# Pooled attention and two feed-forward layers: the first batch in plain fp32 with one order of stages per engine, two buffers for q, x0 loads two places later

## The reference

```
q, k, v: (8, 8, 576, 64)                       # batch, heads, sequence, head size
k_p, v_p = mean of 8 neighbouring keys, values  # 72 of each
attn = softmax(q @ k_p.T / 8)                  # 576 x 72 for each head
x0 = (attn @ v_p), heads side by side           # 4608 x 512
h = x0 @ w1_in;  g = max(0.01 h, h);  x1 = g @ w1_out     # 512 -> 2048 -> 512
h = x1 @ w2_in;  g = h * clip(h + 3, 0, 6) / 6;  out = g @ w2_out
```

## Time and profile before

| | |
|---|---|
| runs, us | 1729.87, 1733.42, 1739.12 (median 1733.42) |
| the profiled execution, us | 1732.34 |
| its span, us | 1730.6 |
| mean granted clock of TensorE | 0.992 |
| busy: PE, DVE, ACT, POOL | 98%, 59%, 37%, 23% |
| DMA | 366.83 MB, mean 212 GB/s |

### The profile page before, as it was taken

How to read it: one execution, slowest core, us unless ns; L and a number is a source line. 1 busy time by engine, 2 the same in 40 slices (tenths; PEclk the granted TensorE clock), 3 DMA queues, 4 the chain that set the end, 5 groups by cost and what they waited for, 6 DMA issues and landing times. The chain is left out here.

```text
span 1730.6 us, 33189 instructions
## 1 busy us (share of the span) xinstructions
PE 1691.3 (98%) x10588; PEld 1506.7 (87%) x10588; DVE 1024.0 (59%) x1807; ACT 632.5 (37%) x1329; POOL 394.1 (23%) x427
## 2 busy tenths in 40 slices
PE   7999999999999999999999999999999999999999
PEld 6788888988888888899999888989898888989898
DVE  7767776686766867666454655454544444444444
ACT  4554443333333433333222333333333333333332
POOL 6226542021120212103332202121211112121200
PEclk8999999999999999999999999999999999999999
DMA  7756877667676676767777757575757675757562
GB/s 199 228 159 201 271 249 247 214 201 259 204 243 220 208 247 215 242 196 268 239 258 245 257 172 224 176 220 175 218 170 220 178 219 171 223 173 223 173 197 77
DMA packets 215810, 366.83 MB, mean 212 GB/s; under 512 B 22464, under 2 KB 47040, under 8 KB 215744
## 3 DMA queue, kind: packets, MB, share of 16 engines
q1 hardware_dynamic: 215744, 366.04, 67.3%
HBM read 308.28 MB, written 57.67 MB: 211 GB/s over the span
## 5 line engine op out<-in xcount | busy, mean ns | idle before, releaser
L1416 PE MATMUL ps_h<-xs_hi,ring 128*128 128x256 f32 x3808 | 823.8, 285 | 20.5 <-ACT p L1045 15.9
L1416 PEld LDWEIGHTS ps_h<-xs_hi,ring 128*128 128x128 f32 x3808 | 645.5, 190 | 69.5 <-ACT p L1045 19.8
L1416 PE MATMUL ps_h<-xs_lo,ring 128*128 128x256 f32 x1904 | 537.4, 282 | 0.0
L1416 PEld LDWEIGHTS ps_h<-xs_lo,ring 128*128 128x128 f32 x1904 | 361.2, 190 | 27.0
L931 ACT ACTIVATE g_hi<-gate 128x512 fp32r<-128x512 f32 x288 | 181.9, 632 | 404.6 <-DVE gate L1126 221.8
L1185 DVE TENSOR_TENSOR u<-ps_h,p 128x256 f32<-128x256 f32 x272 | 114.2, 420 | 205.9 <-PE ps_h L1416 155.0
L1369 PE MATMUL ps_y<-g_hi,wout_hi 128*128 128x512 f32 x576 | 229.2, 398 | 0.5 <-DVE y_stage L1181 0.3
L1370 PE MATMUL ps_y<-g_lo,wout_hi 128*128 128x512 f32 x576 | 228.7, 397 | 0.0
L1370 PE MATMUL ps_y<-wout_lo,g_hi 128*128 128x512 f32 x576 | 227.8, 395 | 0.0
L1369 PE MATMUL ps_y<-wout_hi,g_hi 128*128 128x512 f32 x576 | 227.5, 395 | 0.1
L1371 PE MATMUL ps_y<-g_hi,wout_lo 128*128 128x512 f32 x576 | 226.1, 393 | 0.0
(11 more groups left out here) (115 smaller groups left out, 2021.4 us busy)
## 6 DMA issues: line engine op xcount, KB each, us to landing
ring<-w_in_split SPq DMA_DIRECT2D x920, 256.0 KB, 2.8
w_in_split<-ring SPq DMA_DIRECT2D x56, 256.0 KB, 3.6
w_in_split<-stage SPq DMA_DIRECT2D x56, 256.0 KB, 4.3
k_raw<-in_kT SPq DMA_DIRECT2D x32, 288.0 KB, 3.4
q_raw<-in_qT SPq DMA_DIRECT2D x32, 288.0 KB, 3.1
v_raw<-in_v SPq DMA_DIRECT2D x32, 288.0 KB
x0T<-x_stage SPq DMA_DIRECT2D x32, 288.0 KB, 4.4
x1T<-y_stage SPq DMA_DIRECT2D x36, 256.0 KB, 3.8
```

The lines of the kernel that those rows point to most:

```text
L1416: mm = pe.matmul(banks[BANK_OF[r]], a, b[:, r, c, :], start=r in OPENS and c == 0 and n == 0, stop=c == 1 and n == 2, skip_group_check=True)
```

## The change

The first batch gets an order for each engine (`FIRST_DVE`, `FIRST_ACT`, `FIRST_PE`). PE's order holds tile 0's first block products (`upper` is `first_part(0, 1, chunk)`, `lower` is `first_part(0, 0, chunk)`), so `first_step(0)` on PE keeps only its attention places. DVE sums all four k; POOL's `sum_k` goes. The p·v products of the first batch are plain fp32: POOL writes the sums of v to `v_f`, ACT copies the transposed probabilities to `pT_f`, and `v_sum`, `v_lo` and `pT_lo` fall away there. The second half of unit 3 uses unit 0's bank and `pT_f`. Identity products go to places of PE's own list, into whichever bank is idle. Unit 0 has two q buffers, used in turn from batch 1 on, so that the load waits for the scores of a unit earlier. The lists of places for loads of units (first tile) and of x0 move.

```diff
-X_PLACES = (18, 30, 42, 53)
+X_PLACES = (20, 32, 44, 53)
-FIRST_LOAD_PLACES = (6, 19, 30, 41)
+FIRST_LOAD_PLACES = (4, 18, 29, 40)
-FIRST_X_PLACES = (22, 33, 44, 54)
+FIRST_X_PLACES = (24, 35, 46, 54)
-FIRST_STAGES = [...]
+FIRST_DVE = [("sum_k", 0), ("sum_k", 1), ("scores", 0), ("scores", 1), ("sum_k", 2),
+             ("normalize", 0), ("divide", 0), ("scores", 2), ("sum_k", 3), ("normalize", 1),
+             ("divide", 1), ("scores", 3), ("normalize", 2), ("divide", 2), ("normalize", 3),
+             ("divide", 3), ("split_x", 0), ("split_x", 1), ("split_x", 2), ("split_x", 3)]
+FIRST_ACT = [("place_k", 0), ("place_k", 1), ("exp", 0), ("exp", 1), ("place_k", 2),
+             ("turn_p0", 0), ("exp", 2), ("pv0", 0), ("place_k", 3), ("round", 0),
+             ("turn_p1", 0), ("turn_p0", 1), ("pv1", 0), ("exp", 3), ("round", 1), ("pv0", 1),
+             ("turn_p1", 1), ("turn_p0", 2), ("split_x", 0), ("round", 2), ("pv1", 1),
+             ("pv0", 2), ("turn_p1", 2), ("turn_p0", 3), ("split_x", 1), ("pv1", 2),
+             ("turn_p1", 3), ("split_x", 2), ("pv0", 3), ("round", 3), ("pv1", 3),
+             ("split_x", 3), ("round", 4), ("round", 5), ("round", 6), ("round", 7)]
+FIRST_PE = [("scores", 0), ("scores", 1), ("scores", 2), ("turn_p0", 0), ("pv0", 0),
+            ("scores", 3), ("turn_p1", 0), ("pv1", 0), ("turn_p0", 1), ("pv0", 1),
+            ("turn_p1", 1), ("turn_p0", 2), ("pv1", 1), ("pv0", 2), ("turn_p1", 2),
+            ("turn_p0", 3), ("pv1", 2), ("turn_p1", 3), ("upper", 0), ("pv0", 3), ("upper", 1),
+            ("pv1", 3), ("upper", 2), ("lower", 0), ("lower", 1), ("lower", 2), ("upper", 3),
+            ("lower", 3)]
-WARM_STAGES = {("place_k", 0): 0, ("place_k", 1): 3, ("scores", 0): 5, ("place_k", 2): 4,
-               ("turn_p0", 0): 8, ("pv0", 0): 5}
+WARM_STAGES = {("scores", 1): 4, ("scores", 2): 11, ("pv0", 0): 3, ("scores", 3): 5,
+               ("turn_p1", 0): 1, ("pv1", 0): 3, ("pv0", 1): 3, ("turn_p1", 1): 2,
+               ("pv0", 2): 2, ("turn_p1", 2): 2, ("pv1", 2): 1}
...
-            u.q_raw = buf("q_raw", [P, 2, HALF])
+            u.q_raw = [buf(f"q_raw{i}_", [P, 2, HALF]) for i in range(1 if c else 2)]
+            u.v_f = buf("v_f", [KEYS, 2, P])
+            u.pT_f = buf("pT_f", [KEYS, 2, HALF])
+        def q_of(b, c):
+            return buffers(b, c).q_raw[0 if first(b) else c % 2]
+        def half_buffers(b, c, half):
+            return units[0] if first(b) and c == PAIRS - 1 and half == 1 else buffers(b, c)
...
-                above_zero(sp, scores_done, 2 * freed(b, c))
-                sp.dma_start(u.q_raw[:], qT[b, c]).then_inc(q_loaded[c], 16)
+                if not first(b):
+                    sp.wait_ge(scores_done, 2 * (freed(b, c) - 1))
+                sp.dma_start(q_of(b, c)[:], qT[b, c]).then_inc(q_loaded[c], 16)
...
 # POOL
-                    nc.gpsimd.tensor_tensor(u.v_hi[:, hd, hd * D:(hd + 1) * D],
+                    nc.gpsimd.tensor_tensor(u.v_f[:, hd, hd * D:(hd + 1) * D],
                                             raw_v[:, hd, :, 0], raw_v[:, hd, :, 1], ALU.add
-                                            ).then_inc(v_hi_ready, 1)
-                nc.gpsimd.tensor_tensor(u.v_sum[:], raw_v[:, :, :, 0], raw_v[:, :, :, 1],
-                                        ALU.add).then_inc(v_summed, 1)
-                pool.wait_ge(v_summed, c + 1)
-                v_lo(0, c)
+                                            ).then_inc(v_ready, 1)
+                pool.wait_ge(v_ready, 2 * c + 2)
+                pool.sem_inc(v_summed, 1)
...
-            sum_k(2, 0)
-            sum_v(0, 2)
-            sum_k(3, 4)
-            sum_v(1, 6)
-            sum_v(2, 8)
-            sum_v(3, 10)
+            for c in range(PAIRS):
+                sum_v(c, 2 * c)
...
 # ACT, turn_p0 and turn_p1
-                    nc.scalar.activation(u.pT_hi[:], u.ps[0:KEYS, :, 0:HALF], ACT.Copy
+                    to = at.pT_f if first(b) else at.pT_hi
+                    nc.scalar.activation(to[:], at.ps[0:KEYS, :, 0:HALF], ACT.Copy
...
 # PE, first_part
                 if i == 0:
+                    pe.wait_ge(x0_copied, 4)
                     pe.wait_ge(first_x_ready, chunk + 1)
...
 # PE, pv0 and pv1
+                    if first(b):
+                        pe.wait_ge(pT_hi_ready, half + 2 * n + 1)
+                        for hd in range(2):
+                            mm = pe.matmul(at.ps[:, half, 0:HALF], u.v_f[:, hd, :],
+                                           at.pT_f[:, hd, :], start=hd == 0,
+                                           stop=hd == 1)
...
 # PE, the first batch
+            for name, c in FIRST_PE:
+                if name in ("upper", "lower"):
+                    first_part(0, int(name == "upper"), c)
+                else:
+                    if (name, c) == ("turn_p1", 0):
+                        pe.wait_ge(shifted, 4)
+                        idle = ps_h[:, 0]
+                    if (name, c) == ("turn_p0", 1):
+                        idle = ps_att[:, 0]
+                    keep_warm(WARM_STAGES.get((name, c), 0), idle)
                     stage(name, 0, c)
```

More of the change, by code:

```diff
@@ L536, in _ @@
             sp.wait_ge(scores_done, 2)
-            sp.dma_start(units[0].q_raw[:], qT[1, 0]).then_inc(q_loaded[0], 16)
+            sp.dma_start(q_of(1, 0)[:], qT[1, 0]).then_inc(q_loaded[0], 16)
             store_x0(0, 0)
@@ L655, in _ @@
         def _(pool):
[L656 to L666, removed]
             def sum_v(c, folds):
@@ L971, in stage @@
                                     16 * (b + 1) if c else 16 * b)
-                    nc.scalar.activation(u.x0_stage[:, half, :], u.ps[:, half, 0:HALF],
-                                         ACT.Copy, scale=V_SCALE).then_inc(x0_copied, 1)
+                    nc.scalar.activation(u.x0_stage[:, half, :],
+                                         half_buffers(b, c, half).ps[:, half, 0:HALF], ACT.Copy,
+                                         scale=V_SCALE).then_inc(x0_copied, 1)
             def round_v(b, c):
@@ L1070, in _ @@
             act.wait_ge(kT_zeroed, PAIRS)
-            for name, c in FIRST_STAGES:
+            for name, c in FIRST_ACT:
                 if name == "round":
@@ L1332, in _ @@
                 dve.memset(u.kT[:], 0.0).then_inc(kT_zeroed, 1)
[L1333 to L1335 removed]
+            for name, c in FIRST_DVE:
+                stage(name, 0, c)
             for i in range(HF):
@@ L1459, in stage @@
                     half = int(name[-1])
+                    at = half_buffers(b, c, half)
                     pe.wait_ge(prob_ready, 2 * n + half + 1)
+                    if at is not u:
+                        pe.wait_ge(x0_copied, 2)
                     for hd in ((0, 1), (1, 0))[half]:
-                        if half == 1 and hd == 0:
+                        if half == 1 and hd == 0 and at is u:
                             pe.wait_ge(x0_copied, 2 * n + 1)
                         for j in range(HALF_SUB):
-                            mm = pe.transpose(u.ps[0:KEYS, hd, j * ROWS:(j + 1) * ROWS],
+                            mm = pe.transpose(at.ps[0:KEYS, hd, j * ROWS:(j + 1) * ROWS],
                                               u.prob[:, half, 2 * j + hd, :],
@@ L1470, in stage @@
                     half = int(name[-1])
-                    pe.wait_ge(pT_ready, 2 * n + half + 1)
+                    at = half_buffers(b, c, half)
                     if half == 0:
                         pe.wait_ge(v_ready, 2 * n + 2)
-                    for hd in range(2):
-                        mm = product(u.ps[:, half, 0:HALF], (u.v_hi[:, hd, :], u.v_lo[:, hd, :]),
-                                     (u.pT_hi[:, hd, :], u.pT_lo[:, hd, :]), hd == 0, hd == 1)
+                    if first(b):
+                        pe.wait_ge(pT_hi_ready, half + 2 * n + 1)
[4 more added lines that the diff above has]
+                    else:
+                        pe.wait_ge(pT_ready, 2 * n + half + 1)
+                        for hd in range(2):
+                            mm = product(u.ps[:, half, 0:HALF],
+                                         (u.v_hi[:, hd, :], u.v_lo[:, hd, :]),
+                                         (u.pT_hi[:, hd, :], u.pT_lo[:, hd, :]),
+                                         hd == 0, hd == 1)
                     mm.then_inc(pv_done, 1)
@@ L1487, in place @@
                         stage(name, 1, c)
+                if i == 0:
+                    for m in range(HF):
+                        place(m)
+                    return
                 first_part(i, 1, 0)
@@ L1554, in _ @@
             pe.wait_ge(zeroed, 2)
-            keep_warm(WARM_UP)
-            pe.wait_ge(v_zeroed, 2 * PAIRS)
+            keep_warm(WARM_UP, ps_y[:, DC - 1])
+            pe.wait_ge(v_zeroed, PAIRS + 2)
             pe.wait_ge(kT_zeroed, PAIRS)
-            for i, (name, c) in enumerate(FIRST_STAGES):
```

(10 more changed lines are left out.)

31 lines of the change are left out of this document (12 added, 19 removed).

## The result

The changed kernel takes 1706.98 us (median of four runs, 1705.58 to 1708.51) against 1734.09 (four runs, 1729.87 to 1739.12): a ratio of 0.9843, with a 95% interval of 0.9815 to 0.9871. 1706 had been forecast. The profiled execution took 1708.51 us, with a span of 1706.7; that is 23.9 us less than the span of before, where the medians differ by 27.1.

A forecast was written before the change was run, and what follows sets the result against it. PE, busy 1691.3 of 1730.6 us, bounds the kernel, so gains lie in its idle time and low clock. 8.3 (first batch, net) + 12.0 + 6.7 (tiles) = 27.0 us, giving 1706 on the median's scale; range 1700 to 1710.

The forecast's parts named there:

- The tiles: Attention tiles T = 2 to 6: PE's waits for ACT's copy `p` shrink, 12.0 us, and four clock falls go, 6.7.
- no fall of the clock: Behind the stalls of T = 2 to 6: all four falls of PE's granted clock vanish, 6.7 us, bounds 3.4 and 6.7.
- the store's landing: First `stage2` store in a tile: lands in 4.8 us as before, so 2.9 of 3.1 us come back.
- The first batch: Start of the run: `first_step(1)` on PE starts at 42.3 us instead of 52.14, 9.8 us; ends 6 and 12.
- PE's tail: PE's work from the first half of the last division, 30.6 us, to `first_step(1)` at 42.3.
- The 31.2: First batch on DVE: the last division ends at 31.2 us instead of 35.4; bounds 28.9 and 31.9.
- E: Rival: the orders don't shorten the first batch, one list waiting for another, while the tiles gain: 1714 us; chance 0.04.
- B: Rival: the clock falls in the new prologue too, behind waits for divisions, costing about 6 us: 1712 us; chance 0.12.
- The second step: `first_step(1)`: DMA is late, ACT stands up to 4.4 us for `raw(2)`; 1.5 us charged, bounds 0 and 6.

The follow-up runs named there:

- tiles_only: Kernel before with two q buffers and all moved place lists, the first batch as before: 1714.16 us (0.9877).
- q_only: Kernel before with the two q buffers alone, all place lists and the first batch as before: 1715.46 us (0.9882).
- no_warm: Changed kernel without the 37 identity products between the stages of the first batch (the 8 at the start stay): 1716.77 us (0.9887).
- sp_early: v_ahead with block A12 rounded behind p·v 2 instead of 3 and raw(2) loaded right behind the block stores: 1705.12 us (0.9832).
- v_ahead: Changed kernel with SP's load of v for unit (1, 0) ahead of the stores of x0 and of the blocks: 1705.54 us (0.9829).
- first_only: Changed kernel with one q buffer and the place lists of before, so only the first batch is changed: 1728.53 us (0.9959).

## Why the prediction was right

**The tiles, 18.7 us forecast, 20.2 in the profile, 20.8 by tiles_only.** Each step held: q behind k, x0 store 5.2 us ahead of its load, `stage2`'s store right behind PE's last part (287.27 - 286.38 = 0.9 us after its start; forecast 290.5 - 290.0), no fall of the clock. That the second q buffer is nearly enough follows from the working (the x0 store lands at 288.0, before SP's place 20 at 288.7), and q_only's 19.5 of 20.8 us show it; the moved loads alone give 13.4. One term was mis-sized: I kept the store's landing at 4.8 us and so left 0.3 us in each tile. It went out 2.5 us earlier and not 2.9, set against PE, but landed in 290.83 - 287.27 = 3.6 us. The same store took 4.9 us in q_only, where SP had stood at x0 and then issued that load and three ring loads in the 2 us ahead of it, against that load and one ring load here. That this makes the difference is argued, not shown. The Trainium skill (DMA: Bandwidth & Descriptors, "Anatomy of one DMA") fits a fixed 2.0 us plus bytes over 436 GB/s to transfers that GpSimd issues; SP issues those here. The estimate by it, 2.6 us for 256 KB, is 1.0 us under the measured 3.6, so it is no guide to these stores.

**The first batch, 9.8 us forecast, 8.9 measured.** The last division was forecast for 31.2 and ended at 31.05; the second step for 42.3, and it started at 43.3. The missing 1.0 us is PE's tail, 12.2 us from the last division's end where I had 11.1. A p·v in plain fp32 takes 18.11 - 17.07 = 1.04 us, as taken, and no copy on ACT held PE up: a window of PE over the tail shows it busy throughout.

```profile
31.00:43.25 12.25, 12.25 (x72) 1.00 0.77 245
```

PE came late to it. I had it free for unit 3's transposes when the first half of the last division was done, at 30.6; by its timeline it still had a p·v of unit 2, two identity products and six transposes to do, and reached them near 32.0. From there to the second step are 11.3 us of work without a wait, against 11.0 of work and 0.7 for copies in the sum. So the term that was mis-sized is PE's backlog, of which the working had put the identity products at up to 1.5 us and counted half.

The 31.2 was a hit by two errors that cancel. The four divisions together took 1.7 us less than before (2.36, 1.46, 1.66 and 1.12 against 1.33, 2.31, 2.58 and 2.08 us), where 0.7 had been taken; and one small step of normalizing, `row_den`, took 1.23 us beside a fold of POOL at 20.20, where it takes 0.17 in the other three units. The 1.33 us that the prediction calls alone stood partly beside a fold too; alone it is 1.12.

That the batch isn't shortened (E) is out by the ledger, though what the orders have in it was not separated. B is out by the clock; no_warm shows that B was close, and that the identity products were why it didn't come. By the Trainium skill (SBUF — State Buffer, "Who interferes with whom") a DVE instruction with two inputs in SBUF and a GpSimd instruction that reads SBUF shut each other out. The traces agree: in sp_early divisions took 2.62 and 2.20 us beside POOL's folds and 1.12 without one.

**The second step, 1.5 us forecast, 3.2 measured.** This step failed in its mechanism too. The text had SP stand at the store of block A12 until 35.5 (it was 37.9) and named `raw(2)` as what is late, with ACT standing at it. ACT never waited for `raw`: it came to that rounding only at 50.71, behind two pieces of w_out and the exponentials. Late was the v of unit (1, 0), in the same queue behind the same block store, on DVE in front of the gate (the activation of the feed-forward). v_ahead moves that one load and halves PE's wait. Of all transfers behind a stand of SP the first to be asked for counts, and I had taken the largest.

**Not forecast:** 1.9 us lost between the first tile and the stall of T = 2, part of it in every kernel of the table. Its cause is open. **In total** 27.0 us were forecast for the profile and 23.9 came, 1.7 from the second step, 1.9 before T = 2 and 1.0 from PE's tail, against 1.5 more from the tiles. The medians differ by 27.1, because of where the two profiled executions lie among their runs. So the hit to 1 us is partly luck; the sum's own error was 3 us.

## What to carry to other kernels

An in-order queue of transfers turns a wait for one buffer into a wait for everything behind it: look at what stands at the head when the late transfer could have gone, and free that, by a second buffer or a later place. When TensorE is made to wait for 2 to 3 us, count the lower clock behind the wait as well; here it was a third of what the stalls cost (6.7 of 19.8 us). Where three engines share a chain, try the parts also by taking them out of the whole: fp32 and the identity products gave 3.3 us each alone, and without either one the new order gained nothing.

## What the hardware showed that I had not expected

In no_warm PE stood at half clock from 26 to 48 us although it was busy for 21.96 of these 22. The wait just before was only 0.83 us, at 24.9, and in the 8 us from 18 to 26 PE had been busy for 5.7 with no wait over 1.02. Twice before the clock had been low (0.50 from 12 to 14 us, 0.54 from 20 to 22) and had come back within a few us. With the identity products (37, at 0.21 us) it was at 1.00 throughout. In the kernel before, the clock came back within some 6 us after a wait of 3.1.

A long wait doesn't always bring the clock down. The wait of 3.07 to 3.10 us was followed by a fall in one tile and by none in another. And in the first tile PE waited 3.37 us for the first difference of w_out in the changed kernel and 2.75 in first_only, where PE's list of products is the same. Windows behind these waits, first in the changed kernel,

```profile
50.00:54.00 4.00, 4.00 (x19) 1.00 1.05 383
```

then in first_only:

```profile
50.00:54.00 4.00, 4.00 (x11) 0.50 1.05 397
```

The shorter wait was followed by the fall. So what a wait costs in clock isn't settled by its length, and one profile of each kernel doesn't tell what else decides.
